# Attention, mixture of experts and Mish layer on one core: sorted rows transposed for the second expert alone, and the rest a turn later

## The chip, the core and the metric

The kernel runs on one core of a Trainium2 chip. The metric is device microseconds of one execution, lower is better. The engines are named as in the profile: PE is TensorE (PEld its weight loads), ACT is ScalarE, DVE is VectorE, POOL is GpSimd, SP is SyncE, which here only issues transfers. A name with a q behind it (SPq, PEq) is the engine's sequencer.

## What is computed

768 tokens pass through three layers, all in float32 in and out.

```python
# 1. attention, 8 heads of 64, masked to equal hash buckets (6 bits)
mask = q_bucket[:, :, :, None] == k_bucket[:, :, None, :]
attn_out = softmax(where(mask, scale * q @ k.T, -1e9)) @ v
# 2. mixture of experts: 8 experts, capacity 192, one expert per token
logits = x @ w_gate;  expert_idx = argmax(logits);  gate_w = softmax(logits)[expert_idx]
h = maximum(disp @ w1[e], 0)          # 512 -> 1024
y = h @ w2[e]                         # 1024 -> 512
out[token] = gate_w * y[slot of the token]
# 3. h * tanh(log1p(exp(h))), h = x @ w_in (512 -> 2048), then @ w_out (2048 -> 512)
```

With the inputs of this case the eight experts get 74, 76, 131, 118, 76, 79, 93 and 121 tokens. The third is the only one above 128.

## The kernel before

The program runs in three stages. Attention comes first, 48 units of 128 queries; it ends near 131 us. Then every token gets an expert and a slot, so that the tokens of one expert stand together ("sorted rows"). The experts stage follows, a loop of eight turns (`Fori(0, E)`, L948), one per expert. The Mish stage (L1088 and L1113) takes the rest. Each engine runs its own copy of the loop and waits on semaphores.

**One turn.** A turn of PE multiplies the expert's first weights (`wa`, the memory called `ring` in the profile) with transposed rows (`xs`, 512 features in four parts kd, a column per slot), in `first_layer` (L951, matmuls L959). It then multiplies the result with the second weights, split into a high and a low part (L1006). With at most 128 tokens it runs `narrow` (L992), 128 columns; with up to 144 `wider(MIDDLE)` (L1011). Which one runs is decided by a branch on the expert's count. Inside the first layer, behind the first block fc = 0, PE transposes the rows that the turn before has made (`turn_rows`, L982, matmuls L987), for which ACT has to have evicted `ysb` (L1314). The second weights are split during the turn: ACT rounds a quarter (`w2hi`, L1310), DVE subtracts (`w2lo`, L1647), four times.

**Where the rows come from.** For the first turn a matmul with a one-hot matrix (`hot`, L935) gathers the first expert's rows straight into PSUM banks 4 to 7, transposed; ACT (L1284) and DVE (L1620) evict them into `xs`. For all other turns POOL scatters all rows to `rows` in HBM in the order of their slots (six indirect DMAs, L665). SP waits for these (L517), reads them back to `xg` in three transfers (L520), and PE transposes them in 24 matmuls at the end of turn 0 (`rows_in`, L970, matmuls L978) into six banks. ACT (L1298) and DVE (L1634) evict three banks each.

**SP's order.** SP issues its transfers from one instruction stream: the three reads of `xg` first, then in a loop, for each next expert, the two halves of its first weights (L477, when PE has read the old ones, by the count `Hw`) and of its second weights (L481). Each half is 1 MB. `hold` (L412) is a wait, and L415 its line in the profile.

**POOL.** After the scatters POOL waits for all transposes (`xt`, L668) and the end of turn 1 (`Yw`, L669), and then splits the first ten blocks of the Mish weights, into memory that `hot` and `xg` lie in.

Of the kernel before, what the change touches and what calls it, by code (L numbers as in the profile page):

```python
# [31 lines left out]
P = 128  # L32
# [38 lines left out]
def attention_moe_mish(nc, kt, qt, vt, first, proj1, projs, foldw, w1, w2, w_in, w_out, cf, cb, out,  # L71
# [30 lines left out]
    with ExitStack() as ctx:  # L102
# [37 lines left out]
        mark = place("mark", [P, 5], F32)  # L140
# [53 lines left out]
        hot = place("hot", [P, NT, NARROW], F32)  # L194
        xg = place("xg", [P, NT, DM + 1], F32)
# [62 lines left out]
        for n in ["first_" + n for n in MISH_A + MISH_B] + ["wm" + str(f) for f in range(NS, KFF, 2)] + ["still", "c0", "c", "cr", "k0", "q00", "q01", "k1", "q1", "pj", "pj2", "qs", "cl", "passed_sp", "passed_gp", "rk0", "rk1", "rv0", "rv1", "ca", "cq", "cp", "pja", "pjb", "ah", "ab", "ao", "ak", "aq", "ka", "kl", "ks", "ch", "cc", "opsA", "opsB", "wa0", "wa1", "wb0", "wb1", "wi", "wo", "wi2", "wo2", "out",  # L258
                  "pjh", "pjl", "wg",
                  "S", "max", "P", "T", "hi", "lo", "PV", "OT", "os", "om", "xw", "fw", "fr", "lx", "lr", "pa", "pd", "vs", "rc", "tiny",  # L260
                  "g", "gex", "ohm", "lth", "gt", "gm", "gpos", "gst", "gkr", "hotr", "xga", "xgd", "perm", "tokc", "tokr", "prime", "si", "sc", "back", "back2", "wide", "xw0", "xw1", "xt", "xa", "xd",
# [11 lines left out]
        TURN = 4  # L273
# [53 lines left out]

        def load_bounds(engine, e):
# [7 lines left out]
        SHORT = WIDE // NEAR  # L336
        YB, YT, SLOW = 4, (5, 4), 6
        assert LAST_IN + 2 * NS + KF == 2 * KFF
        XT_BANKS = (0, 1, 2, 3, SLOW, SLOW + 1)
        FIRST_ROWS = 4  # L340
        assert FIRST_ROWS % NEAR == 0 and SHORT <= P
# [62 lines left out]
        def wide_slots(ks):  # L404

            return xs[:, ks, 0:WIDE].rearrange("q k (p t) -> q k t p", t=NEAR)

        def wide_tiles(bank):

            return ps[:, bank, 0:2 * WIDE].rearrange("q (k t p) -> q k t p", k=2, t=NEAR)  # L410
# [7 lines left out]
        def _(sp):  # L418
# [120 lines left out]
        def _(gp):  # L539
# [103 lines left out]
            nc.gpsimd.memset(mark[:, 0:1], 0.0).then_inc(s["xa"], 1)  # L643
            nc.gpsimd.memset(mark[:, 1:2], 0.0).then_inc(s["xd"], 1)
            nc.gpsimd.memset(mark[:, 2:3], 0.0).then_inc(s["Ha"], 2)
            nc.gpsimd.memset(mark[:, 3:4], 0.0).then_inc(s["Hd"], 2)
            nc.gpsimd.memset(mark[:, 4:5], 0.0).then_inc(s["ye"], 2)
# [20 lines left out]
            gp.wait_ge(s["xt"], 6)  # L668
# [22 lines left out]
        def _(pe):  # L691
# [238 lines left out]
            for t, kd in order:  # L930
# [4 lines left out]
                last = mm(ps[:, 4 + kd, 0:NARROW], xq[:, t, 2 * kd:2 * kd + 2, :].rearrange("p h d -> p (h d)"),  # L935
# [3 lines left out]
            pe.wait_ge(s["bnd"], 1)  # L939


            pe.wait_ge(s["bnd"], 1)
# [5 lines left out]
            with pe.Fori(0, E) as e:  # L948
                st, n_e = (pe.snap(x, min_val=0, max_val=T) for x in (at_r, many_r))

                def first_layer(W, fcs):  # L951

                    for fc in fcs:
                        if fc % (KF // 2) == 0:
                            pe.wait_ge(s[f"wa{2 * fc // KF}"], 16 * (e + 1))
                        for kd in range(KD):
                            if fc == 0:
                                pe.wait_ge(s["xd" if kd % 2 else "xa"], TURN * e + 2 + kd // 2)
# [3 lines left out]
                                      start=(kd == 0), stop=(kd == KD - 1), skip_group_check=True)  # L962
                        if fc % 2:
                            last.then_inc(s["Hw"], 1)

# [4 lines left out]
                def rows_in():  # L970

                    pe.wait_ge(s["back"], 16 * FIRST_ROWS // NEAR)
                    for b in XT_BANKS:
                        if b == SLOW:
                            pe.wait_ge(s["back2"], 16)
# [4 lines left out]
                        last.then_inc(s["xt"], 1)  # L980
# [11 lines left out]
                def narrow():  # L992

                    first_layer(NARROW, range(1))
                    turn_rows(e + 1)
                    first_layer(NARROW, range(1, KF))
# [14 lines left out]
                def wider(W):  # L1011

                    first_layer(W, range(1))
                    turn_rows(e + 1)
                    first_layer(W, range(1, KF))
# [16 lines left out]
                    with pe.If(e < 1):  # L1032
                        pe.wait_ge(s["ya"], 4)
                        pe.wait_ge(s["yd"], 4)
# [8 lines left out]
                with pe.If(e < 1):  # L1043
                    rows_in()
# [3 lines left out]
            with nc.body("pe_more", parent=turn, valid_engines=[pe.engine]):  # L1048
                with pe.If(e < 1):
                    pe.wait_ge(s["xa"], 3)  # L1050
                    pe.wait_ge(s["xd"], 3)
                    pe.wait_ge(s["back"], 16 * FIRST_ROWS // NEAR)
                    for kd in range(KD):
                        for t in range(NEAR):
                            at = WIDE * (kd % 2) + SHORT * t
                            last = mm(ps[:, 4 + kd // 2, at:at + SHORT], xg[0:SHORT, t, P * kd:P * kd + P],
                                      c32("ident")[0:SHORT, 0:SHORT], is_transpose=True, start=True, stop=True)
                    last.then_inc(s["wide"], 1)
                    pe.wait_ge(s["xw0"], 1)
# [734 lines left out]
```

## Time and profile before

| | us |
|---|---|
| median of 3 runs | 396.7 (396.29 to 397.35) |
| the profiled execution, its time | 397.59 |
| the profiled execution, its span | 395.8 |
| PE busy in it | 384.1 (97%) |
| attention and sorting, to the first turn | 0 to 141.2 |
| the eight turns | 141.2 to 256.3 |
| the Mish stage and the output | 256.3 to 395.8 |

The span is what the trace covers, and the execution's own time is 1.8 us more. PE is busy nearly all the time, so what PE waits for, and the clock it is granted, decide the time. A timeline row gives start, duration, engine, line and operation, out<-in and the count of instructions merged; square brackets hold the idle time before it and what ended it. Rows of PE overlap their neighbours because matmuls are pipelined. PE's count is two per matmul of float32 in the first layer (64 for 32 matmuls).

### The profile page before, as it was taken

The numbers are of one execution on the slowest core, as the hardware profiler recorded it, in microseconds if no ns is written. First come the engines' busy times: TensorE is split into PE (matmuls) and PEld (weight loads), VectorE is DVE, ScalarE is ACT, GpSimd is POOL, SyncE is SP. The second block draws the span as 40 slices with busy tenths as digits, with TensorE's granted clock in tenths as the row PEclk, the third lists the DMA queues.
The fourth block names the chain that finished last, engine by engine and source line by source line (L and its number), as shares of the span: only waits on it lengthen the run. The fifth ranks groups of instructions, "written<-read, shape, count | busy, mean of one in ns | idle before, by whom it ended". The sixth has DMA issues, their size and how long they took to land.

```text
span 395.8 us, 6807 instructions
## 1 busy us (share of the span) xinstructions
PE 384.1 (97%) x2384; PEld 348.2 (88%) x2386; DVE 281.6 (71%) x446; ACT 235.2 (59%) x454; POOL 116.1 (29%) x122
## 2 busy tenths in 40 slices
PE   8999999999999998899999999999999999999994
PEld 3688999999999897899998999899899988999883
DVE  4888998899998644430447744569899998876851
ACT  6969879869887544430444654467666665444631
POOL 1853543643810250039999400000000000000014
PEclk9999999999999999899999999999999999999999
DMA  8684934974903347896798889090000000000004
GB/s 284 227 200 106 268 82 131 291 152 111 417 34 146 127 159 292 332 368 238 263 365 286 296 333 357 0 317 5 0 2 0 2 0 2 1 0 2 0 4 162
DMA packets 16124, 62.93 MB, mean 159 GB/s; under 512 B 3008, under 2 KB 3904, under 8 KB 11488
## 3 DMA queue, kind: packets, MB, share of 16 engines
q1 hardware_dynamic: 14560, 58.61, 43.9%
q0 software_dynamic: 1024, 3.22, 2.2%
q10 hardware_dynamic: 512, 0.73, 0.5%
q8 instruction: 17, 0.28, 0.3%
q14 instruction: 11, 0.09, 0.1%
HBM read 49.89 MB, written 3.22 MB: 134 GB/s over the span
## 4 chain that ended last, share of the span: by engine, by line
PE 58%; DMA 3%; POOL 1%; issue 0%; SPq 0%; POOLq 0%; ACT 0%; DVE 0%; ACTq 0%
PE ps L1088 17%; PE ps L1113 16%; PE ps L959 13%; PE ps L1006 8%; DMA ring<-in_w 2%; PE ps L1027 2%; DMA rows<-xg,sloti 1%; PE ps L987 1%; POOL rows L665 0%; SPq L520 0%; POOLq L102 0%; POOL out L687 0%; DVE outs L1751 0%; ACT yh L1320 0%; ACT ysb L1314 0%
## 5 line engine op out<-in xcount | busy, mean ns | idle before, releaser
L959 PE MATMUL ps<-xs,ring 128*128 x512 | 61.9, 280 | 2.4 <-DMA ring<-in_w 2.4
L959 PEld LDWEIGHTS ps<-xs,ring 128*128 128x128 f32 x512 | 60.8, 195 | 3.1 <-issue 2.7
L1555 DVE TENSOR_TENSOR ptl<-ps,pth 128x384 fp32r<-128x384 f32 x96 | 49.0, 552 | 4.3 <-ACT pth L1246 3.7
L1246 ACT ACTIVATE pth<-ps 128x384 fp32r<-128x384 f32 x96 | 41.9, 491 | 16.0 <-PE ps L881 15.7
L1478 DVE TENSOR_REDUCE nmax<-ps 128x1 f32<-128x768 f32 x48 | 45.7, 955 | 4.9 <-PE ps L751 2.0
L683 POOL DMA_INDIRECT spare<-fold,toki x1 | 1.0, 1009 | 161.4 <-PE ps L1113 161.4
L751 PE MATMUL ps<-ops 128*128 128x384 f32 x192 | 44.4, 353 | 0.8 <-DMA ops<-qo 0.7
L1200 ACT ACTIVATE prob<-ps,nmax 128x768 f32<-128x768 f32 x48 | 43.5, 906 | 0.2 <-DVE nmax L1478 0.2
L1088 PE MATMUL ps<-yh,wih 128*128 128x384 f32 x128 | 43.0, 336 | 0.3 <-ACT yh L1320 0.3
L1088 PE MATMUL ps<-yh,wlow 128*128 128x384 f32 x128 | 42.8, 335 | 0.0
L1088 PE MATMUL ps<-yl,wih 128*128 128x384 f32 x128 | 41.9, 335 | 0.0
L1647 DVE TENSOR_TENSOR w2lo<-ring,w2hi 128x1024 fp32r<-128x1024 f32 x28 | 37.5, 1338 | 4.9 <-ACT w2hi L1310 4.7
L881 PE MATMUL ps<-cfs,prob 128*128 128x128 f32 x288 | 39.9, 273 | 0.7 <-DVE ptl L1555 0.7
L1113 PE MATMUL ps<-woh,gl 128*128 128x512 f32 x96 | 37.6, 392 | 0.0
L1113 PE MATMUL ps<-wlow,gh 128*128 128x512 f32 x96 | 37.6, 391 | 0.0
L881 PEld LDWEIGHTS ps<-cfs,prob 128*128 128x128 f32 x288 | 33.9, 140 | 4.0 <-DVE ptl L1555 2.1
L1113 PE MATMUL ps<-woh,gh 128*128 128x512 f32 x96 | 37.3, 389 | 0.0
L751 PEld LDWEIGHTS ps<-ops 128*128 128x128 f32 x192 | 33.6, 189 | 2.4 <-issue 1.7
L853 PE MATMUL ps<-pth,vs 128*128 128x384 f32 x90 | 34.2, 379 | 0.0
L1372 ACT ACTIVATE et<-ps 128x768 f32<-128x768 f32 (+1 forms) x19 | 13.4, 706 | 30.9 <-PE ps L1088 30.9
L853 PE MATMUL ps<-ptl,vs 128*128 128x384 f32 x90 | 30.3, 337 | 0.0
L1310 ACT ACTIVATE w2hi<-ring 128x1024 fp32r<-128x1024 f32 x28 | 29.4, 1050 | 0.1
(192 smaller groups left out, 782.9 us busy)
## 6 DMA issues: line engine op xcount, KB each, us to landing
ring<-in_w SPq DMA_DIRECT2D x32, 1024.0 KB, 4.8
wraw<-in_w_in SPq DMA_DIRECT2D x2, 1280.0 KB, 8.1
wraw<-in_w_out SPq DMA_DIRECT2D x2, 1280.0 KB, 10.8
ops<-kh SPq DMA_DIRECT2D x12, 192.0 KB, 6.0
ops<-qh SPq DMA_DIRECT2D x6, 384.0 KB, 8.2
xg<-rows SPq DMA_DIRECT2D x3, 513.0 KB, 4.9
raw<-in_vt SPq DMA_DIRECT2D x4, 384.0 KB, 5.3
wraw<-in_w_in SPq DMA_DIRECT2D x6, 256.0 KB, 4.4
```

The source lines that it names most:

```text
L751: last = mm(ps[:, b + c, 0:HALF], o[:, a, P * u:P * u + P], o[:, kk, c * HALF:c * HALF + HALF], start=(a == QA), stop=(a == QB), skip_grou ...
L853: last = mm(ps[:, OB, 0:HALF], vs[:, (m // 4) % 2, ch, (m // 2) % 2, :, :].rearrange("p a d -> p (a d)"), x[:, m % 2, ch, :, :].rearrange( ...
L881: last = mm(ps[:, tile_banks(n)[b], P * ch:P * ch + P], prob[:, n % 2, HALF * b + P * ch:HALF * b + P * ch + P], c32("ident"), is_transpos ...
L959: last = mm(ps[:, fc // 2, (fc % 2) * WIDE:(fc % 2) * WIDE + W], wa[:, 2 * fc // KF, kd, P * (fc % (KF // 2)):P * (fc % (KF // 2)) + P], x ...
L1006: last = mm(ps[:, YB, :], x[:, fc, :], w, start=(fc == 0 and n == 0), stop=(fc == KF - 1 and n == 2))
L1088: last = mm(ps[:, bank + c, 0:HALF], w[:, kd, :], y[:, kd, c * HALF:c * HALF + HALF], start=(n == 0), stop=(n == 3 * KD - 1))
L1113: last = mm(ps[:, t, :], g[:, f % 4, ts], w, start=(first and n == 0), stop=(final and n == 2), skip_group_check=True)
L1200: av(prob[:, n % 2, :].rearrange("p (c n) -> p c n", c=2), score_tile(n), ACT.Exp, bias=nmax[:, n % 4:n % 4 + 1], accum_out=rowsum[:, n:n ...
L1246: av(pth[:, (n // HT) % 2, HT * b:HT * b + HT, n % HT, :], ps[:, tile_banks(n)[b], 0:HALF].rearrange("p (a c) -> p a c", c=P), ACT.Copy).t ...
L1478: V.tensor_reduce(nmax[:, n % 4:n % 4 + 1], score_tile(n), AX.XY, ALU.max, negate=True).then_inc(s["max"], 1)
L1555: V.tensor_tensor(ptl[:, m2, HT * b:HT * b + HT, u, :], ps[:, tile_banks(n)[b], 0:HALF].rearrange("p (a c) -> p a c", c=P), pth[:, m2, HT ...
L1647: V.tensor_tensor(low[:, 2 * (b % 2):2 * (b % 2) + 2, :], wb[:, b // 2, 2 * (b % 2):2 * (b % 2) + 2, :], w2hi[:, 2 * b:2 * b + 2, :], ALU. ...
```

## The change

Between turn 0 and turn 1 only one window of 128 slots is read back and transposed, the one that begins at the second expert's first slot. All sorted rows are read back later, behind the second expert's weights in SP's order, and transposed at the end of turn 1 for turn 2 and those after it. The window's start is a run-time value: DVE computes it (`second_at`, at most 768 - 128), and SP, ACT and DVE load it into a register. The window is read into the memory of `hot`, which is free by then. The gather's banks change from 4, 5, 6, 7 to 4, 3, 6, 7. In the first layer the first two blocks are now multiplied with kd 0 and 1 first, then `turn_rows` comes, then kd 2 and 3 of them, then the other blocks; the waits for `xs` go with these two halves. A branch for a wide second or third expert changes too; with these counts only its `e != 1` branch around `turn_rows` and an empty one are run, in turn 2.

```diff
@@ SP @@
+            sp.wait_ge(s["bnd"], 2)
+            at_second = load_second(sp)
             sp.wait_ge(s["sc"], 16 * NT)
             sp.wait_ge(s["perm"], KD)
-            for g in range(0, NT, NEAR):
+            sp.dma_start(second, rows[bass.ds(at_second, P), 0:DM]).then_inc(s["back"], 16)
+            def sorted_rows(g):
                 sp.dma_start(xg[:, g:g + NEAR, :], rows[P * g:P * g + P * NEAR, :].rearrange(
-                    "(p t) x -> p t x", t=NEAR)).then_inc(s["back" if g < FIRST_ROWS else "back2"], 16)
+                    "(p t) x -> p t x", t=NEAR)).then_inc(s["back2"], 16)
...
                     second_weights(i + 1, half)
+                if i == 0:
+                    for g in range(0, NT, NEAR):
+                        sorted_rows(g)
@@ POOL @@
-            gp.wait_ge(s["xt"], 6)
+            gp.wait_ge(s["xt"], 2 + len(REST_BANKS))
@@ PE @@
+                def first_layer(W, turned=False):
+                    pe.wait_ge(s["wa0"], 16 * (e + 1))
+                    pe.wait_ge(s["xa"], e + 1)
+                    pe.wait_ge(s["xd"], e + 1)
+                    layer_part(W, range(2), range(KD // 2))
+                    if turned:
+                        with pe.If(e != 1):
+                            turn_rows(e + 1)
+                    else:
+                        turn_rows(e + 1)
+                    pe.wait_ge(s["xa"], TURN * e + 2)
+                    pe.wait_ge(s["xd"], TURN * e + 2)
+                    layer_part(W, range(2), range(KD // 2, KD))
+                    layer_part(W, range(2, KF // 2), range(KD))
+                    pe.wait_ge(s["wa1"], 16 * (e + 1))
+                    layer_part(W, range(KF // 2, KF), range(KD))
...
+                def second_rows(s_done):
+                    for kd in range(KD):
+                        last = mm(ps[:, SLOW + 2 * kd // KD, P * (kd % 2):P * (kd % 2) + P], second[:, P * kd:P * kd + P],
+                                  c32("ident"), is_transpose=True, start=True, stop=True)
+                        if kd % 2:
+                            last.then_inc(s_done, 1)
...
-                with pe.If(e < 1):
-                    rows_in()
+                with pe.If(e < 2):
+                    with pe.If(e < 1):
+                        pe.wait_ge(s["back"], 16)
+                        second_rows(s["xt"])
+                        pe.wait_ge(s["xd"], TURN + 2)
+                    with pe.Else():
+                        all_rows(s["xt"])
+                        pe.wait_ge(s["xa"], TURN + 3)
+                        pe.wait_ge(s["xd"], TURN + 3)
@@ ACT (DVE alike, with the other half and the banks 0, 6, 3) @@
+                def second_rows():
+                    act.wait_ge(s["xt"], 2)
+                    av(xs[:, KD // 2:KD, bass.ds(at_second, P)], second_tiles(SLOW + 1), ACT.Copy).then_inc(s["xa"], TURN)
+                def all_rows(s_ready, ready, s_part, s_all, many):
+                    for n, b in enumerate(REST_BANKS[1::2]):
+                        act.wait_ge(s_ready, ready + 2 * n + 2)
+                        done = av(many_slots(b), many_tiles(b), ACT.Copy)
...
@@ DVE, before the loop @@
+            V.tensor_scalar(second_at[:, :], ps[:, 2, 1:2], float(T - P), None, ALU.min).then_inc(s["bnd"], 1)
             for t in range(1, NT, 2):
                 V.tensor_scalar(xg[:, t, 0:DM], ...).then_inc(s["xgd"], 1)
+            dve.wait_ge(s["bnd"], 2)
+            at_second = load_second(dve)
```

`TURN` is 2 and `REST_BANKS` is (0, 1, 6, 2, 3, 7): `all_rows` on PE fills these banks in this order with four transposes each, DVE evicts 0, 6, 3 and ACT 1, 2, 7. Banks 0 and 1 and bank 6 hold kd 0 and 1.

## Rows read from the trace of the kernel before

**Rows 1.** The page's first line.

```profile
span 395.8 us, 6807 instructions
```

**Rows 2.** PE's timeline from turn 0 to turn 2's second layer.

```profile
141.16 1.12 PE L959 MATMUL ps<-xs,ring 128*128 x8
...
148.72 0.48 PE L1006 MATMUL ps<-w2hi,hsh 128*128 128x512 f32 x1
...
154.03 0.39 PE L1006 MATMUL ps<-w2hi,hsl 128*128 128x512 f32 x1
154.38 2.84 PE L978 MATMUL ps<-cfs,xg 128*128 128x128 f32 x24
159.66 1.56 PE L959 MATMUL ps<-xs,ring 128*128 x8 [2.44 <-DMA ring<-in_w]
...
168.90 0.48 PE L1006 MATMUL ps<-w2hi,hsh 128*128 128x512 f32 x1
...
174.46 1.14 PE L959 MATMUL ps<-xs,ring 128*128 x8
...
182.74 8.00 PE L1027 MATMUL ps<-hs,ring 128*128 128x144 f32 x64
```

**Rows 3.** PE's timeline, the beginnings of turns 5 and 6.

```profile
216.94 1.05 PE L959 MATMUL ps<-xs,ring 128*128 x8
...
230.01 1.05 PE L959 MATMUL ps<-xs,ring 128*128 x8
```

**Rows 4.** SP's timeline: issues of transfers, three reads first, then weights.

```profile
149.04 1.28 SPq L520 DMA_DIRECT2D xg<-rows  x3
150.44 1.11 SPq L477 DMA_DIRECT2D ring<-in_w  x2
151.79 0.82 SPq L481 DMA_DIRECT2D ring<-in_w  x2
165.66 3.90 SPq L477 DMA_DIRECT2D ring<-in_w  x2
```

**Rows 5.** DMA issues, size, us to landing: at 149.0, 150.4, 152.3 and 165.7.

```profile
xg<-rows SPq DMA_DIRECT2D x1, 513.0 KB, 3.7
...
ring<-in_w SPq DMA_DIRECT2D x1, 1024.0 KB, 9.0
...
ring<-in_w SPq DMA_DIRECT2D x1, 1024.0 KB, 14.5
...
ring<-in_w SPq DMA_DIRECT2D x1, 1024.0 KB, 4.8
```

**Rows 6.** Stretches: length, PE, PEld, DVE, ACT, POOL busy, granted clock, DMA share, GB/s.

```profile
151.00:152.00 1.00, 1.00 (x7) 0.81 (x6) 0.59 (x1) 0.00 (x0) 0.00 (x0) 1.00 0.92 365
...
157.00:158.00 1.00, 0.22 (x3) 0.00 (x0) 0.75 (x2) 0.50 (x1) 0.00 (x0) 1.00 1.05 442
...
161.00:162.00 1.00, 1.00 (x7) 1.00 (x6) 0.00 (x0) 0.23 (x1) 0.00 (x0) 0.50 1.08 459
...
256.00:257.00 1.00, 0.53 (x4) 0.20 (x2) 0.00 (x0) 0.65 (x2) 0.00 (x0) 1.00 0.00 0
```

**Rows 7.** Timelines of ACT and DVE: evictions and splits around turn ends.

```profile
154.46 0.66 ACT L1314 ACTIVATE ysb<-ps 128x256 f32<-128x256 f32 x2 [4.12 <-PE ps L1006]
...
177.65 0.41 ACT L1329 ACTIVATE hs<-ps 128x288 f32<-128x288 f32 x1 [1.05 <-PE ps L959]
...
150.37 1.23 DVE L1647 TENSOR_TENSOR w2lo<-ring,w2hi 128x1024 fp32r<-128x1024 f32 x1 [0.23 <-ACT w2hi L1310]
155.51 0.69 DVE L1634 COPY xs<-ps 128x512 f32<-128x512 f32 x1 [3.92 <-PE ps L978]
```

**Rows 8.** Groups by form on DVE: count, busy, mean ns of one.

```profile
L1654 DVE TENSOR_TENSOR yl<-ps,yh 128x256 f32 x14 | 5.4, 421 | 30.9 <-ACT yh L1320 30.9
```

**Rows 9.** DVE's scaling before the loop, and POOL's second scatter.

```profile
137.65 1.27 DVE L1616 TENSOR_SCALAR xg<-xq,gk 128x512 f32<-128x512 f32 x3
...
139.35 0.96 POOL L665 DMA_INDIRECT rows<-xg,sloti  x1 [0.30 <-issue]
```

More of the change, by code:

```diff
@@ L326, in wait_task_read, with load_second @@
                 e.wait_ge(s["pa"], PA * (g - 1) + t - 4 + 1)
+        def load_second(engine):
+            return nc.values_load_multi_w_load_instructions(
+                second_at[0:1, 0:1], engines=(engine.engine,), min_val=0, max_val=T - P,
+                skip_runtime_bounds_check_because="at most T - P by the minimum that is written there")[1][0]
         def load_bounds(engine, e):
@@ L402, in many_tiles, with second_tiles @@
             return ps[:, b, :].rearrange("q (k t p) -> q k t p", k=2, p=P)
[L404 to L410, printed above, removed]
+        def second_tiles(bank):
+            return ps[:, bank, 0:2 * P].rearrange("q (k p) -> q k p", k=2)
         def hold(e, passed, semaphore, value):
@@ L992, in narrow @@
                 def narrow():
[L994 to L996 removed]
+                    first_layer(NARROW)
                     pe.wait_ge(s["ya"], 2 * e + 2)
@@ L1011, in wider @@
                 def wider(W):
-                    first_layer(W, range(1))
-                    turn_rows(e + 1)
-                    first_layer(W, range(1, KF))
+                    first_layer(W, True)
                     pe.wait_ge(s["ya"], 2 * e + 2)
@@ L1048, in _ @@
             with nc.body("pe_more", parent=turn, valid_engines=[pe.engine]):
[L1049 to L1059, printed above, removed]
-                    pe.wait_ge(s["xw1"], 1)
+                with pe.If(e < 2):
+                    with pe.If(e < 1):
+                        pe.wait_ge(s["xa"], 2)
+                        pe.wait_ge(s["wide"], 16)
+                        for kd in range(KD):
+                            last = mm(ps[:, SLOW, P * kd:P * kd + P], xg[:, 0, P * kd:P * kd + P], c32("ident"),
+                                      is_transpose=True, start=True, stop=True)
+                        last.then_inc(s["xwt"], 1)
+                        pe.wait_ge(s["wider"], 1)
+                    with pe.Else():
+                        turn_rows(e + 1)
+                        pe.wait_ge(s["xa"], TURN + 2)
+                        all_rows(s["xr"])
+                        pe.wait_ge(s["xra"], 1)
+                        pe.wait_ge(s["xrd"], 1)
                 pe.br_cond(n_e < MIDDLE + 1, "pe_middle", "pe_wide")
@@ L1292, in _ @@
                 st, n_e = load_bounds(act, e)
-                def rows_in():
-                    for n, b in enumerate(XT_BANKS[0::2]):
-                        act.wait_ge(s["xt"], 2 * n + 1)
-                        av(many_slots(b), many_tiles(b), ACT.Copy).then_inc(
-                            s["xa"], 1 if b < SLOW else TURN * (E - 2) + 2)
+                def second_rows():
[5 more added lines that the diff above has]
+                        done = av(many_slots(b), many_tiles(b), ACT.Copy)
+                        if n == 0 and s_part is not None:
+                            done.then_inc(s_part, 1)
+                        if n == 2:
+                            done.then_inc(s_all, many)
+                def rows_in():
+                    with act.If(e < 2):
+                        with act.If(e < 1):
+                            second_rows()
+                        with act.Else():
+                            all_rows(s["xt"], 2, s["xa"], s["xa"], ALL_TURNS - TURN - 3)
                 def narrow():
```

116 lines of the change are left out of this document (63 added, 53 removed).

## The prediction, as it was made before the changed kernel ran

> **What bounds the kernel now.** I read the page first, then PE's timeline through the turns, and then, for the one place where PE stands still, what the transfers and the clock do there. The span is 395.8 us [rows 1]. PE runs from turn to turn without a hole, and a steady narrow turn takes 230.01 - 216.94 = 13.07 us [rows 3]; turn 0 takes 154.38 - 141.16 = 13.22 us up to its transposes [rows 2]. The exception lies between turn 0 and turn 1. After 24 transposes PE idles 2.44 us, and what ends it is a transfer into `ring`, the first half of the second expert's first weights [rows 2]. It was issued at 150.44, behind the three reads of sorted rows (149.04), and needed 9.0 us; the same transfer on idle queues needs 4.8 us [rows 4, 5]. In the stretches shown the DMA engines are 0.92 to 1.08 busy, at 365 to 459 GB/s [rows 6]. So the weights wait for 1.5 MB of rows, of which turn 1 reads a sixth, 128 of 768 slots.
>
> A second loss follows. PE's granted clock is 1.00 in the pause and 0.50 at 161 to 162, that is 1.2 GHz and not 2.4 [rows 6]. Turn 1's first layer takes 168.90 - 159.66 = 9.24 us where turn 0's takes 148.72 - 141.16 = 7.56 us [rows 2]: 1.68 us lost. From the first transpose (154.38) to turn 2's first matmul (174.46) pass 20.08 us [rows 2]. This stretch is what the change works on.
>
> **The stretch with the change, step by step.** (1) SP issues a read of 128 rows of 2 KB, 0.26 MB, at 149.04, since the scatters that it waits for stay. The first 513 KB read landed after 3.7 us [rows 5], so this one is there by 152.7 at the latest, and PE asks for it at 154.38. It costs nothing, with 1.7 us of cover.
>
> (2) The first weights go out two issues of about 0.45 us earlier, near 149.5. An idle queue gives 149.5 + 4.8 = 154.3 [rows 5]; 0.26 MB ahead of them at 365 GB/s [rows 6] is 0.7 us if nothing of it overlaps, so 154.3 to 155.0. The halves behind follow at 2.5 us each: from the first half's landing at 159.4 to the fourth's at 152.3 + 14.5 = 166.8 are three halves [rows 4, 5]. That puts the other three near 157, 159.5 and 162.
>
> (3) PE transposes four tiles in place of 24, and now waits for DVE's copy of the first two. Before, DVE's first copy began 155.51 - 154.38 = 1.13 us after the first transpose, behind eight of them [rows 2, 7]. A transpose takes 2.84 / 24 = 0.118 us [rows 2]; six fewer make 0.43 us. The copy has 128x256 elements, for which the nearest group of DVE shows 0.42 us [rows 8]. ACT's copy of the other half begins when its `ysb` evictions end, at 155.12 [rows 7], and is needed only behind the first four matmuls and `turn_rows`; it is covered. Sum: 0.85 us.
>
> (4) Behind this wait stand PE's own branches: two ends of conditionals, the loop's end, the choice of the path. Until now they ran under matmuls still queued; now PE's queue is empty. From below the cost is nothing: at 154.38 a conditional left only some 0.12 us between the last matmul (154.03, one every 0.23) and the first transpose [rows 2]. From above it is the 1.05 us that ACT sat between its last eviction of turn 1 and its first of turn 2, with the loop's end, a register load and three branches in it [rows 7]; ACT, not the matmul, was late there. PE's way has no load from memory behind the wait, so I take 0.4. Turn 1 then starts at 154.38 + 0.85 + 0.4 = 155.6, and its weights (154.3 to 155.0) are there. The Trainium skill (Advanced Engine Details and Errata, Control Flow Timing) gives about 51 ns for a plain branch and 108 ns for a compare-and-branch. No row here isolates one; the estimate from that page would be 0.3 to 0.5 us, so it would leave the sum where it is.
>
> (5) Turn 1 costs 13.2 us, like turn 0, if the clock holds. Its splits need the second weights in time. Turn 0's last split ends at 151.60, 2.9 us behind the second layer's start [rows 2, 7]; a quarter of the second layer is (154.38 - 148.72) / 4 = 1.4 us, so PE needs it at +4.2: slack 1.3 us. In turn 1 the second layer starts at 163.2. The fourth half lands at 162; two roundings and two subtractions of 1.05 to 1.23 us behind it end near 166.4, against a need at 167.4. The cover is 1.0 us.
>
> (6) At the end of turn 1 (168.8) come the 24 transposes that have moved. They aren't cheaper than before, but dearer: before, they ran while the weights were under way anyway, and now nothing hides their 2.8 us. PE then waits for DVE's second copy and ACT's first. DVE's third bank of transposes is there 1.6 us after the first, its copy takes 0.69 [rows 7], so the wait ends at 2.3 us, and with 0.4 of branches at 2.7: under the transposes. With 1.05 of branches it would be 3.35, or 0.55 more. The other copies end about 3.5 us in, while PE does four matmuls and `turn_rows` (0.9 + 0.45 us); nothing.
>
> (7) The three reads now follow the fourth half (162). At 300 to 400 GB/s, 1.58 MB end at 166 to 167.3; needed at 168.8. Turn 2's first weights are issued near 160.2, queue behind them and land at 168.6 to 169.9; needed at 171.6. The cover is 1.5 us on both. Turn 2's second weights are needed only at the second layer, 8.3 us later [rows 2].
>
> (8) Small things, at nothing: DVE's added minimum (about 0.2 us) stands ahead of the scalings that POOL's scatters wait for, but DVE begins them at 137.65 and POOL takes the second at 139.35, bound by its own issue [rows 9]. The register loads stand where SP, ACT and DVE wait anyway. POOL's splits of Mish weights begin when turn 1's last copies are done, so beside turn 2, as before. The matmuls and waits per turn are as many as before, in another order. Behind turn 2 everything hangs on PE and moves along.
>
> **Sum:** 20.08 - (0.85 + 0.4 + 13.2 + 2.8) = 20.08 - 17.25 = 2.8 us gained. With the ends of step 4 (nothing, or 1.05 twice) it is 1.6 to 3.3. In other words: 2.44 of waiting and 1.68 of half clock go, and 1.3 come back as a new pause.
>
> The profiled execution took 397.59, 0.9 above the median of 396.7. Against itself it would give 394.8, against the median 393.9. Part of the runs' spread may be that not every run pays the half clock; then the median has less to win. I take 394.2.
>
> **The rivals.** (A) The pause in front of turn 1 still brings the clock down. It lasts about 0.8 us against 2.44. For: one pause of 2.44 did it. Against: in 256 to 257 PE was busy for only 0.53 us and kept 1.00 [rows 6]. Price 1.7: 395.9. Chance 0.12. (B) One of the covers of 1.0 and 1.5 us in steps 5 and 7 is too thin, since the transfers of two stages now follow without a break; 1 us is lost: 395.2. Chance 0.10. (C) The stall only moves: turn 2's first weights land 2.4 us after the need, at 174, and the half clock comes with it, as before. Price 2.4 + 1.7 = 4.1: 398.3. It decides from a mean rate under 300 GB/s over the 7.1 MB since 150.4; the trace shows 5.8 MB landed by 166.8, 350 GB/s, slow reads included. Chance 0.05. (D) Slower: the first weights don't come earlier, because the reads were not what held them. Then turn 1 starts at 159.66 with the half clock as before, and the 2.8 us of step 6 are added without anything in return: 399.5. The point at which gain turns to loss is a start of turn 1 at 174.46 - 16.0 = 158.4. Against: 9.0 against 4.8 us for the same transfer. Chance 0.03.
>
> (E) The changed loop body leaves PE without code at one of the added branches, and the code comes through busy queues, at most like a weight transfer, 4.8 us: 399.0. In the trace no branch of the loop shows such a gap, but the code there is laid out otherwise. Chance 0.02. The Trainium skill (Runtime: NRT & Kernel Launch, Instruction fetch mechanics) says that a taken branch out of the two pages held stalls the engine until the target page is fetched; that speaks against added branches in the loop, and no row here shows such a stall.
>
> **How the numbers follow.** My forecast has 0.68, and the likeliest time is 394.2. Its own range is 393.3 (3.3 off the median) to 395.6. The range reaches over B and most of A to 396.3; C, D and E, 0.10, stay out. A measurement of this kernel can tell 0.3%, 1.2 us, from no change, so faster means under 395.5. Nearly all of the forecast and of B, and some of A: 0.80. The rest of A and B, and a small part of the forecast: 0.11. C, D, E: 0.09.
>
> **What would show it.** PE's turn 1 should start near 155.6, with an idle of about 0.8 us before it put down to DVE's copy (step 3, 4), not to a transfer into `ring`; if it is over 1.5, the branches cost more than the upper end. Clock 1.00 from 155 to 165 and a first layer of about 7.6 us (step 5). 24 transposes near 168.8, turn 2 at about 171.7, no idle before it (6, 7). A wait for `ring` or `xg` at either place is B or C. The prediction is wrong in its core if the first weights land after 156, or if later turns take over 13.1 us each.

## The result, and the profile after

The kernel got slower: 401.03 us median of five executions (399.28 to 402.03) against 396.5 (396.29 to 397.35), ratio 1.0104, interval 1.0082 to 1.0127. The forecast was 394.2 with a range up to 396.3. The five fall into two groups. Two have a mean granted clock of 0.999 and take 399.3 and 399.9 us; three have 0.994 or 0.995 and take 401.0 to 402.0. The profiled execution is the first, 399.28 with a span of 397.5, against 395.8 in [rows 1]. One later execution, of early_three, took 641.61 us at a mean granted clock of 0.558, where its nine others took 393.6 to 395.2, and no time or count below includes it.

PE's timeline of the changed kernel (start, busy us, line, operation, count, idle before and what ended it), which answers to [rows 2]:

```profile
141.26 1.13 PE L967 MATMUL ps<-xs,ring 128*128 x8
...
156.04 0.60 PE L999 MATMUL ps<-cfs,hot 128*128 128x128 f32 x4
158.66 1.15 PE L967 MATMUL ps<-xs,ring 128*128 x8 [2.02 <-issue]
...
171.82 2.78 PE L1010 MATMUL ps<-cfs,xg 128*128 128x128 f32 x24
175.86 1.24 PE L967 MATMUL ps<-xs,ring 128*128 x8 [1.25 <-ACT xs L1342]
```

There are three places to see. Turn 0 lasts 156.04 - 141.26 = 14.78 us, where it lasted 13.22. Before turn 1 stands an idle of 2.02 that no transfer ends, and before turn 2 one of 1.25 that wasn't there. Turn 1 itself takes 171.82 - 158.66 = 13.16.

The chain of work that ended last, in order of time, at both pauses:

```profile
156.20 0.45 PE ps L999 x4
156.65 0.26 issue
156.91 0.44 DVE xs L1694
157.35 1.31 issue
158.66 1.15 PE ps L967 x8
...
171.98 2.63 PE ps L1010 x24
...
174.70 0.64 ACT xs L1342
175.34 0.52 issue
175.86 1.24 PE ps L967 x8
```

DVE's copy ends at 157.35 and PE's first matmul comes 1.31 us later, with "issue" between them: the weights lie there, and nothing that the profile records is waited for. What PE's queue does in between is recorded line by line (line, engine, operation, duration in ns three times, start and end in us). Among eight control instructions are three compare-and-branches, at the end of the conditional (L1072), at the loop's end (L960) and at the choice of the path (L1066):

```profile
L1072 PEldq COMPARE_BRANCH  x1: 194/194/194, 157.4 to 157.4; - x1
L960 PEldq COMPARE_BRANCH  x1: 220/220/220, 157.7 to 157.7; - x1
L1066 PEldq COMPARE_BRANCH  x1: 68/68/68, 158.1 to 158.1; - x1
```

The other five are register and semaphore instructions of 36 to 80 ns, and none of the eight starts more than 0.2 us after the end of the one before. So the 1.31 us are a row of small instructions, and no single stall. At the second pause the chain names ACT's last copy, but the waits in the code are for ACT's first copy and DVE's second, and DVE's second is the later one:

```profile
173.33 0.69 DVE L1700 COPY xs<-ps 128x512 f32<-128x512 f32 x1 [0.18 <-PE ps L1010]
```

It ended at 173.33 + 0.69 = 174.02. Behind it stand five compare-and-branches. SP's issues, answering to [rows 4], and the landings, answering to [rows 5]:

```profile
149.20 0.35 SPq L527 DMA_DIRECT2D hot<-rows  x1
149.67 0.83 SPq L483 DMA_DIRECT2D ring<-in_w  x2
...
ring<-in_w SPq DMA_DIRECT2D x1, 1024.0 KB, 5.0
hot<-rows SPq DMA_DIRECT2D x1, 256.0 KB, 2.8
```

The read landed at 152.0 and the first weights at 149.67 + 5.0 = 154.7, both 1.3 us or more before turn 0 was over. The transfers did what the prediction said of them. The loss is elsewhere.

For the experiments I divide the stretch from turn 0's first matmul to turn 2's first matmul, by PE's timeline. From turn 2's first matmul to the end of the span it is 221.5 or 221.6 us in the profiles of the changed kernel, 221.0 or 221.1 in those with the waits inside, and 221.3 and 221.0 in the two of before. In us ("to turn 1" and "to turn 2" are the transposes and the pause behind them; where turn 1's part is 14.8, turn 1 ran partly at half clock, that is a granted clock of 0.50, 1.2 GHz):

| kernel | turn 0 | to turn 1 | turn 1 | to turn 2 | whole |
|---|---|---|---|---|---|
| before [rows 2] | 13.22 | 5.28 | 14.80 | 0 | 33.30 |
| after | 14.78 | 2.62 | 13.16 | 4.04 | 34.60 |
| again | 13.15 | 2.52 | 13.15 | 4.04 | 32.86 |
| waits_inside | 13.17 | 2.30 | 13.67 | 2.62 | 31.76 |
| before_again | 14.89 | 3.20 | 13.58 | 0 | 31.67 |
| again_two | 14.77 | 2.53 | 14.80 | 4.08 | 36.18 |
| inside_two | 14.63 | 1.07 | 13.15 | 2.62 | 31.47 |
| again_three | 13.16 | 2.61 | 13.14 | 4.07 | 32.98 |
| early_three | 13.18 | 1.07 | 13.15 | 2.62 | 30.02 |

### The profile page after: what moved, and what is told of

The parts are those of the page before. It is cut to its first block, busy times and chain, and to the rows that moved or that the text cites. A ratio compares the mean times of both kernels' runs of the same rounds, so it can differ in the third digit from the quotient of the medians.

```text
span 397.5 us, 6844 instructions
## 1 busy us (share of the span) xinstructions
PE 383.4 (96%) x2389; PEld 346.6 (87%) x2390; DVE 282.2 (71%) x448; ACT 234.7 (59%) x455; POOL 116.1 (29%) x120
## 4 chain that ended last, share of the span: by engine, by line
PE 88%; DVE 3%; ACT 3%; issue 2%; DMA 2%; POOLq 0%; POOL 0%; SPq 0%; ACTq 0%; DVEq 0%
PE ps L1126 17%; PE ps L1151 16%; PE ps L967 14%; PE ps L1036 9%; PE ps L865 7%; PE ps L763 7%; PE ps L893 7%; PE ps L1055 2%; PE ps L720 2%; PE ps L947 1%; PE ps L836 1%; ACT prob L1238 1%; PE ps L1019 1%; DMA eproj<-in_proj 1%; ACT pth L1284 1%
## 5 line engine op out<-in xcount | busy, mean ns | idle before, releaser
L967 PE MATMUL ps<-xs,ring 128*128 x512 | 60.7, 276 | 3.3 <-issue 2.0
L967 PEld LDWEIGHTS ps<-xs,ring 128*128 128x128 f32 x512 | 59.4, 191 | 4.1 <-issue 3.7
```

The lines of the kernel that those rows point to most:

```text
L967: last = mm(ps[:, fc // 2, (fc % 2) * WIDE:(fc % 2) * WIDE + W], wa[:, 2 * fc // KF, kd, P * (fc % (KF // 2)):P * (fc % (KF // 2)) + P], x ...
```

## The experiments

They ran in four batches of four kernels, each with its own runs of before. Two theories stood at first. By the first, PE's branches behind a wait that blocks cost what is missing. By the rival, it is what else is new: the order of work (the banks and the split first layer), or the loads of the second expert's address.

**First batch.** before took 396.18 here.

**again**: the changed kernel, no edit.

> The changed kernel once more, for a second trace. In its first trace turn 0 takes 14.78 us instead of 13.22, because ACT's first eviction of turn 0 (hsh) begins at 146.66, 2.9 us behind the matmuls that it waits for. If that comes from the code, ACT's idle time ahead of its first hsh is over 5 us again and turn 0 again takes 14.5 to 15 us. If it was chance, ACT begins near 143.8 and turn 0 takes 13.2 us. Either way PE should stand 1.3 us between the end of DVE's copy and turn 1's first matmul, and 1.2 us ahead of turn 2. Ratio to before 1.007 to 1.013.

Measured: 397.52, ratio 1.0046 (1.0026 to 1.0066). Slower again, but by 1.3 us and not by 4.5. Turn 0 took 13.15, and the pauses were the same two. So the pauses are the kernel's own; turn 0's extra 1.6 us is not.

**waits_inside**: PE's waits for the copies no longer stand at the turn's end, ahead of its branches, but in the next turn's first layer, on counters of their own.

```diff
@@ PE, first layer @@
-                    pe.wait_ge(s["xa"], e + 1)
-                    pe.wait_ge(s["xd"], e + 1)
+                    pe.wait_ge(s["xpa"], e + 1)
+                    pe.wait_ge(s["xpd"], 3 * e + 1)
...
@@ PE, end of turns 0 and 1 @@
                         second_rows(s["xt"])
-                        pe.wait_ge(s["xd"], TURN + 2)
                     with pe.Else():
                         all_rows(s["xt"])
-                        pe.wait_ge(s["xa"], TURN + 3)
-                        pe.wait_ge(s["xd"], TURN + 3)
...
```

> The waits for the evictions stand in the first layer of the turn that needs them, on counters of their own, and no longer at the end of the turn before; so PE's branches run while its matmuls still drain. Theory (the pauses are branches laid bare by a wait ahead of them): 1.3 us less in front of turn 1 and 1.2 us less in front of turn 2, so about 2.5 us faster than the changed kernel, ratio to before 1.001 to 1.007; if the half clock comes from the longer pause, it goes too and the ratio is below 1.0. Rival (the pauses are the copies and the transfers themselves): no change, the idle time is then put down to a copy, and the ratio stays at 1.010.

Measured: 395.2, ratio 0.9964 (0.9943 to 0.9986). 2.3 us below again, for the same work in the same order. The pause before turn 2 is gone (4.04 to 2.62, the bare transposes), and the one before turn 1 is now ended by the weights, by the chain of waits:

```profile
149.31 6.96 DMA ring<-in_w
156.28 0.22 issue
156.49 1.15 PE ps L967 x8
```

The transfer took 7.0 us here where it took 5.0 in the first profile. Turn 1 itself is 0.5 longer than in again, for the second weights are late too: ACT's first rounding of them in turn 1 waits for the transfer.

```profile
161.25 1.06 ACT L1362 ACTIVATE w2hi<-ring 128x1024 fp32r<-128x1024 f32 x1 [1.55 <-DMA ring<-in_w]
```

This kernel is no faster than before at full clock. Of the 22 executions of before in this batch the eight with a mean clock over 0.996 have a median of 395.1.

**old_order**: the first layer's old order and banks, with the moved reads kept.

```diff
-        GATHER = (4, 3, SLOW, SLOW + 1)
+        GATHER = (4, 5, SLOW, SLOW + 1)
...
-                    layer_part(W, range(2), range(KD // 2))
+                    pe.wait_ge(s["xa"], TURN * e + 2)
+                    pe.wait_ge(s["xd"], TURN * e + 2)
+                    layer_part(W, range(1), range(KD))
...
```

> The first layer in the old order (block 0 whole, then the transposes of the turned rows, then the rest) and the gather in the old banks 4 to 7; all else as in the changed kernel. Theory (the interleaved order or the new bank makes turn 0's first results late for ACT): turn 0 takes 13.2 us again, ACT begins at 143.8, 1.5 us less. Rival (it comes from the loads of the window's start, or from chance): turn 0 stays at 14.8 us. In front of turn 2 PE now waits for all copies, about 1 us more than the changed kernel.

Measured: 398.66, ratio 1.0063 (1.0042 to 1.0084), 1.1 above again. PE waited for 2.22 and 1.50 us at the two places and started turn 0 with a wait of 0.57 for DVE. The new order isn't the cause; it gains 1.1 us.

**loads_inside**: ACT's and DVE's loads of the second expert's address moved into turn 0's end (DVE's part; ACT's is alike).

```diff
             dve.wait_ge(s["bnd"], 2)
-            at_second = load_second(dve)
...
                 def second_rows():
 
+                    at_second = load_second(dve)
                     dve.wait_ge(s["xt"], 1)
```

> ACT and DVE load the window's start into a register only at the end of turn 0, not ahead of the loop; all else as in the changed kernel. Theory (the added load ahead of the loop makes ACT late in turn 0): ACT's first hsh begins near 143.8, turn 0 takes 13.2 us, 1.5 us less. Rival (the order of the first layer, or chance): turn 0 stays at 14.8 us. The load then stands in front of the copies of the window, where it costs 0.5 us or is hidden by the transposes.

Measured: 397.41, ratio 1.0031 (1.0008 to 1.0053), like again within the error. The rival falls as the cause of the pauses: from the end of DVE's copy (154.92) to PE's first matmul (156.14) it is 1.22 us here too. But the stretch is 32.51 us, 0.35 shorter than in again, since DVE's copy begins 154.50 - 153.99 = 0.51 us after the first transpose and not 0.87:

```profile
154.50 0.42 DVE L1694 COPY xs<-ps 128x256 f32 x1 [3.22 <-PE ps L999]
```

**Second batch.** before took 396.41 here.

**before_again**: before, no edit.

> The kernel before, unchanged, for a second trace of it. The prediction counted 1.68 us of half clock in turn 1 as lost in every run of it. If that holds, turn 1's first layer takes about 9.2 us here too, behind an idle of 2.4 us that a transfer into ring ends, and the later clock is 0.5 for a stretch. The other theory, that only some runs pay it: a first layer of 7.6 us, the same idle of about 2.4 us, and a span shorter by about 1.7 us (394.2). Ratio 1.000 by both.

Measured: 396.35, ratio 1.0001 (0.9988 to 1.0015). Neither of the two courses expected, but a third:

```profile
141.45 0.89 PE L959 MATMUL ps<-xs,ring 128*128 x6
142.96 0.48 PE L959 MATMUL ps<-xs,ring 128*128 x2 [0.63 <-DVE xs L1620]
...
156.34 2.78 PE L978 MATMUL ps<-cfs,xg 128*128 128x128 f32 x24
159.54 1.54 PE L959 MATMUL ps<-xs,ring 128*128 x8 [0.42 <-ACT xs L1298]
...
173.12 1.14 PE L959 MATMUL ps<-xs,ring 128*128 x8
```

Turn 0 is late here too (14.89), turn 1 starts at 159.54 where it started at 159.66 in [rows 2], and the idle has shrunk from 2.44 to 0.42. There is no half clock in these turns, and turn 2 starts at 173.12, earlier than with the short turn 0. So the 2.44 us idle of [rows 2] is slack for turn 0: when turn 0 is late, before loses nothing.

ACT's timeline shows how it is late. Its first eviction of turn 0, in before_again:

```profile
140.75 0.28 ACT L1284 ACTIVATE xs<-ps 128x128 f32<-128x128 f32 x1 [1.51 <-PE ps L935]
146.98 0.38 ACT L1305 ACTIVATE hsh<-ps 128x256 fp32r<-128x256 f32 x1 [5.95 <-PE ps L959]
```

In the profiled execution of before that eviction began at 143.64, after 2.90 of idle; in the changed kernel of the first result at 146.66, after 5.82:

```profile
143.64 0.38 ACT L1305 ACTIVATE hsh<-ps 128x256 fp32r<-128x256 f32 x1 [2.90 <-PE ps L959]
```

```profile
146.66 0.38 ACT L1360 ACTIVATE hsh<-ps 128x256 fp32r<-128x256 f32 x1 [5.82 <-PE ps L967]
...
153.20 0.47 PE L1036 MATMUL ps<-w2hi,hsh 128*128 128x512 f32 x1 [0.77 <-DVE hsl L1718]
```

PE's matmuls run on in the records meanwhile, but ACT sees their results some 3 us later than in the short course. Then DVE and ACT split the second weights late, and PE waits for them in the second layer. By ACT's idle ahead of this eviction, ten of the 18 profiles of this study have the short turn 0 (2.8 to 3.7 us) and eight the late one (5.8 to 6.0), and nothing lies between. The late eight are the first result's profile, all four of the second batch and three of the third.

**before_early**: before, with one issue moved.

```diff
+            hold(sp, s["passed_sp"], s["Hw"], 2)
+            first_weights(1, 0)
             sp.wait_ge(s["sc"], 16 * NT)
...
-                    hold(sp, s["passed_sp"], s["Hw"], 4 * i + 2 * half + 2)
-                    first_weights(i + 1, half)
+                    if i or half:
+                        hold(sp, s["passed_sp"], s["Hw"], 4 * i + 2 * half + 2)
+                        first_weights(i + 1, half)
```

> The kernel before with one issue moved: the first half of the second expert's first weights goes out when the first half of turn 0's first layer is done (near 146.8), ahead of the wait for the scatters and of the three reads; nothing else is changed. If the idle before turn 1 is due to the weights queued behind the reads, and PE's branches cost little there because matmuls cover them, turn 1 starts right behind the 24 transposes (157.2), 2.4 us earlier: about 393.9 against 396.4 (ratio 0.994), and the clock stays at 1.00. If the reads now come late (two of them share the engines with 0.5 MB of weights), the transposes of turn 0's end start up to 1 us later: 394.9.

Measured: 396.27, ratio 0.9998 (0.9980 to 1.0016). Turn 0 was late, the weights were no longer awaited, and nothing was gained: whole stretch 31.86 against 31.67.

**early_inside**: waits_inside with the same issue moved (the same edit of SP).

> waits_inside with the same issue moved: the first weights of turn 1 near 146.8 instead of 149.4. In waits_inside they landed 2 us behind turn 0's end and set turn 1's start at 156.49. If nothing else is late, turn 1 starts when the four transposes (154.7) and DVE's first copy (0.42, after 0.3 of idle) are through: near 155.4, 1.0 us earlier than there, 0.9974 of waits_inside, about 394.2 against 395.2. If PE's branches are still behind the last wait, 156.0 and 394.8.

Measured: 396.05, ratio 0.9991 (0.9977 to 1.0005). Turn 0 took 14.68, to turn 1 1.07, to turn 2 2.61. The pause before turn 1 is as expected, but behind a late turn 0.

**before_warm**: before, with ten matmuls on zeros behind the 24 transposes.

```diff
                     rows_in()
+                    keep_clock(10, 5)
```

> The kernel before with ten matmuls on a tile of zeros (128x512, 0.21 us each, into a free bank) behind the 24 transposes of turn 0's end, so that PE is busy while it waits for the weights; the weights come no earlier. If the half clock is paid in each run of before, this gains 1.7 us (394.7, ratio 0.9957). If the median run of before doesn't pay it, the ratio is 1.000 and only the slowest runs become rarer.

Measured: 396.96, ratio 1.0016 (0.9994 to 1.0039). Turn 0 was late, so little idle was left to fill; the filler delayed turn 1, which began 161.67 - 156.90 = 4.77 us after the first transpose where before_again had 3.20. The run doesn't settle the price of the half clock, since there was none to save.

**Third batch.** before took 395.86 here. The new theory: the changed kernel has lost the slack that hid a late turn 0.

**again_two**: the changed kernel, no edit.

> The changed kernel, unchanged, once more. The traces so far show two courses of turn 0 for both kernels: one of 13.2 us, in which ACT starts its first eviction 2.9 us after its last copy, and a late one of 14.7 to 14.9 us, in which that takes 5.8 to 5.9 us. Theory: before hides the late course, since its turn 1 starts at 159.5 with the weights either way; the changed kernel doesn't. Where the late course comes up in this batch, this takes 399 to 401 (ratio 1.007 to 1.010), turn 0 lasts 14.8 us; where it does not, 397.5 (ratio 1.004 or 1.005) and 13.2 us. If the course has nothing to do with it, the ratio is 1.0046 with either.

Measured: 400.5, ratio 1.0098 (1.0063 to 1.0132), with turn 0 at 14.77. The first result's ratio is back, and the late turn 0 with it. Not only the profiled execution is late: at a mean clock of 0.998 or more, two of the four here took 399.2 and 399.9, where those of again and again_three took 397.0 to 397.8. The profiled execution of this run is one of those with the half clock. PE's timeline, and the stretches (length, busy us of PE, PEld, DVE, ACT, POOL, granted clock, DMA share, GB/s):

```profile
158.89 1.15 PE L967 MATMUL ps<-xs,ring 128*128 x8 [1.92 <-issue]
...
173.69 2.78 PE L1010 MATMUL ps<-cfs,xg 128*128 128x128 f32 x24
177.77 1.24 PE L967 MATMUL ps<-xs,ring 128*128 x8 [1.30 <-ACT xs L1342]
...
159.00:160.00 1.00, 1.00 (x9) 1.00 (x10) 0.00 (x0) 0.00 (x0) 0.00 (x0) 0.97 0.98 410
160.00:161.00 1.00, 1.00 (x7) 1.00 (x6) 0.00 (x0) 0.39 (x2) 0.00 (x0) 0.50 1.08 442
```

The clock falls from 2.4 to 1.2 GHz 1.1 us after the new pause, and turn 1 takes 14.80 where it took 13.16 after a pause of the same length in the first profile: 1.64 us.

**inside_two**: waits_inside, no edit.

> waits_inside, unchanged, once more, to be compared with again_two in one batch. It should be 2.3 us under it as in the first batch if the two pauses behind the copies are what it saves, whichever course turn 0 takes. Against before: 395.2 (0.9964) with the short turn 0, 397 (1.001) with the late one.

Measured: 396.11, ratio 0.9997 (0.9980 to 1.0014). 4.4 us below again_two, more than the 2.3 expected. The chain shows what is left of the pause, 0.12 in place of 1.21 or 1.31 between copy and matmul:

```profile
156.89 0.44 DVE xs L1691
157.33 0.12 issue
157.45 1.15 PE ps L967 x8
```

And the half clock doesn't come up in this kernel: of the 48 executions with the waits inside (this kernel and the early ones) none has a mean granted clock under 0.997, of the 21 of the unedited changed kernel eight have 0.994 or 0.995. The pause's length alone doesn't decide it. waits_inside had 1.70 us of idle in its profile and none of nine, loads_inside 1.56 and one of ten, old_order 2.22 and none of four.

**early_two**: early_inside, no edit.

> early_inside, unchanged, once more, to be compared with inside_two in one batch. Theory: with the short turn 0 the first weights land 2 us behind its end, and issuing them at 146.8 instead of 149.4 brings turn 1 forward by 0.9 to 1.1 us: 394.2 (0.9939 of before). With the late turn 0 they have landed anyway, and the two kernels are equal within 0.4 us.

Measured: 396.12, ratio 1.0001 (0.9991 to 1.0012). Equal to inside_two, as expected with a late turn 0.

**plain_writes**: POOL's indirect writes made direct, so the tokens stay unsorted.

```diff
-                gp.indirect_dma_start(out=rows[:, :], out_offset=bass.IndirectOffsetOnAxis(ap=sloti[:, t:t + 1], axis=0),
-                                      in_=xg[:, t, :], in_offset=None).then_inc(s["sc"], 16)
+                gp.dma_start(rows[P * t:P * t + P, :], xg[:, t, :]).then_inc(s["sc"], 16)
```

> The changed kernel with POOL's six indirect writes of the rows replaced by six direct writes of the same size to unsorted places (it leaves out the sorting of the tokens, so the experts see other rows; the work on them is the same). The late course of turn 0 lies beside these six writes. If they hold back PE's signals, or the start of the kernel's turns, turn 0 lasts 13.2 us here where again_two has 14.8, and the kernel gains about 1.5 us more than the writes' own end brings. If the late course comes from elsewhere, turn 0 is as long as in again_two. Either way SP's read of the second rows goes out up to 3 us earlier, which alone is worth nothing for turn 1's start, since its weights wait for turn 0's first layer.

Measured: 398.21, 2.3 below again_two on the same chip and, at a mean clock of 0.998 or more, 397.4 to 398.6 against 399.2 and 399.9, ratio 1.0052 (1.0034 to 1.0069) to before. Turn 0 took 13.09, and ACT was on time:

```profile
144.72 0.38 ACT L1359 ACTIVATE hsh<-ps 128x256 fp32r<-128x256 f32 x1 [2.87 <-PE ps L966]
```

The four profiles of this batch are three late turns with the indirect writes and one short turn without them. The direct writes are also issued sooner, by 142.4 where the indirect ones take until 145.9 in again_two, so the kind of write and its time aren't told apart.

**Fourth batch.** before took 395.32 here.

**writes_later**: the indirect writes held back until half of turn 0's first layer is done.

```diff
+            gp.wait_ge(s["Hw"], 2)
             for t in range(NT):
```

> The changed kernel with POOL's six indirect writes held back until half of turn 0's first layer is done (Hw 2, near 145), some 7 us later than before. Where turn 0 takes its late course (14.8 us, again_three in this batch) and the writes themselves hold PE's signals, the gather's last copies and turn 0's first layer are on time here (first eviction 2.9 us after ACT's last copy and not 5.9) and the hold, if any, appears later. If it comes from something else at this place, ACT's first eviction is as late as in again_three. The rows then arrive about 6 us late, near 160, so turn 1 starts later and the time is 4 to 6 us above again_three.

Measured: 405.69, ratio 1.0254 (1.0221 to 1.0287), from two executions. Turn 0 was short in again_three as well, so this tells nothing of the late course. The rows came late: PE waited 6.00 us for `hot`.

**again_three**: the changed kernel, no edit.

> The changed kernel, unchanged, as the measure for this batch: 397.5 with the short turn 0 (13.2 us), 400.5 with the late one (14.8 us).

Measured: 397.39, ratio 1.0062 (1.0028 to 1.0096), turn 0 at 13.16. As with again: short turn 0, 397.4.

**early_two_before**: before_early, no edit.

> before_early, unchanged, once more: the kernel before with only the first weights issued ahead of the reads. With the late turn 0 it gave nothing (0.9998). If this batch has the short turn 0, the weights are there when the 24 transposes end, and turn 1 starts 2.0 to 2.4 us earlier than in before, with no half clock: about 394 (ratio 0.994). With the late turn 0 again 1.000.

Measured: 395.07, ratio 0.9982 (0.9961 to 1.0002). With a short turn 0 the earlier weights brought no gain that can be told either, since they took bandwidth from the rows that PE transposes next. Their reads landed after 5.9 us (median) where they took 4.9 in before, and PE waits for them:

```profile
155.88 1.97 PE L981 MATMUL ps<-cfs,xg 128*128 128x128 f32 x16 [1.02 <-DMA xg<-rows]
158.58 1.09 PE L981 MATMUL ps<-cfs,xg 128*128 128x128 f32 x8 [0.74 <-DMA xg<-rows]
160.09 1.47 PE L962 MATMUL ps<-xs,ring 128*128 x8 [0.41 <-ACT xs L1301]
```

So the change's idea, to read only the 128 rows that turn 1 needs, does what it is for: weights early and all rows early don't go together.

**early_three**: early_inside, no edit.

> early_inside, unchanged, once more. With the short turn 0: turn 1 starts about 14.2 us after turn 0 (13.2, four transposes, and a pause of 0.5), turn 2 at 30.0 us after it where waits_inside had 31.8: 393.5 to 394.2 (ratio 0.993 to 0.995). With the late turn 0: 1.000 as in the last batch.

Measured: 394.34, ratio 0.9964 (0.9950 to 0.9978), 3.05 below again_three. PE's timeline:

```profile
154.69 0.60 PE L1002 MATMUL ps<-cfs,hot 128*128 128x128 f32 x4
155.76 1.15 PE L970 MATMUL ps<-xs,ring 128*128 x8 [0.47 <-DVE xs L1694]
...
168.91 2.78 PE L1013 MATMUL ps<-cfs,xg 128*128 128x128 f32 x24
171.53 1.15 PE L970 MATMUL ps<-xs,ring 128*128 x8
```

The whole stretch is 30.02 us, 0.5 below the 30.5 that the prediction's steps give (13.22 + 0.85 + 0.4 + 13.2 + 2.8). This kernel is faster than both where turn 0 is short, and even with before (0.9991, 1.0001) and 4.4 us faster than the changed kernel where it is late. The gain over before in this batch is not the half clock alone: the 18 of 21 executions of before with a mean clock over 0.996 have a median of 395.2.

## Why the prediction was wrong

The steps that concerned transfers were right. Those that concerned PE at a wait, and what before really loses, were not.

By its steps the stretch would have taken 13.22 + 17.25 = 30.47 us. In again_two it took 36.18, 5.71 more: 1.55 in turn 0, 1.28 up to turn 1 (steps 3 and 4), 1.60 in turn 1 (the half clock, rival A) and 1.28 up to turn 2 (step 6). The prediction's sum is a gain of 2.8 and the result a loss of 4.5, 7.3 apart. The 1.6 that are left are the half clock of [rows 2], counted as a loss in before, which most of its executions outside the first batch don't show.

**Steps 1, 2, 5 and 7, right.** The read landed at 152.0 (said: by 152.7), the first weights at 154.7 (154.3 to 155.0). Turn 1 took 13.15 and 13.16 us (13.2) with no wait for the second weights, and no wait for `xg` or `ring` stands before turn 2. Rivals B to E didn't come up in the changed kernel: no transfer was waited for, and PE's control instructions follow each other with no gap over 0.2 us (E). The covers of step 2 and step 5 are thin all the same. In waits_inside the first weights landed at 156.3, past the prediction's own mark of 156, and the second weights cost turn 1 0.5 us.

**Step 4 is the one that failed, for the size.** It took the branches behind the wait at 0.4 us and gave 1.05 as an upper bound, from ACT's branches. They cost 1.31 and 1.21 in the chains, 0.12 with the waits inside, so 1.1 to 1.2 us. A bound from another engine was no bound for PE: its compare-and-branches lasted 194, 220 and 68 ns there, and five more instructions stood between them, which the step didn't count. The Trainium skill (Advanced Engine Details and Errata, Control Flow Timing) has 108 ns for a compare-and-branch, from which I estimated 0.3 to 0.5; the three records and the 1.1 to 1.2 us in all disagree, and the measurement decides.

**Step 3** was short by 0.46: DVE's copy ends 157.35 - 156.04 = 1.31 after the first transpose, not 0.85, since it begins 0.87 after it and not 0.43. With the waits inside it begins 0.51 after it (156.89 - 156.38), and in loads_inside too, where DVE's load of the address is moved. So 0.36 of the 0.46 go with either edit. Why wasn't found. Steps 3 and 4 together: 2.52 to 2.62 against 1.25.

**Step 6 failed where it called the branches hidden.** It let DVE's second copy end at 2.3 us, under the transposes; it ended at 174.02 - 171.82 = 2.20. From there to turn 2's first matmul it is 1.84 us, not 0.4. Even the version with 1.05 was too small. 4.04 against 2.8, so 1.2 more; waits_inside takes them all back (2.62).

**The sum was made against a loss that before doesn't always have.** The prediction credited 1.68 us for the half clock and asked itself whether all runs pay it. In the first batch 14 of 22 executions of before have a mean clock of 0.996 or less; in the three others 10 of 75. And where turn 0 is late, the idle of 2.44 isn't there: before_again, 31.67 us and full clock. (Seven of the 54 executions of before in the two batches with late profiles still have 0.996 or less; no trace shows where.) Against 31.6 to 31.7 the changed kernel's 32.9 is 1.2 us of loss, and up to 0.5 more lies behind turn 2's first matmul (221.5 us against 221.0 to 221.3). In the medians, 397.52 - 396.18 and 397.39 - 395.32 are 1.3 and 2.1.

**What the prediction didn't have at all** is the late turn 0. It took the 2.44 us of idle as a loss to be won. It is also the cover for a turn 0 that is about 1.6 us late in eight of 18 profiles. Take it away, and the lateness shows: 2.9 us over before_again in the first profile (34.60 - 31.67), and 4.5 with the half clock in again_two (36.18 - 31.67). In terms, for three of the first result's five executions, with before_again standing for before and again_two for the half clock: turn 1 starts 17.4 us after turn 0 in place of 18.1 (-0.7), it is itself 0.4 shorter than in before_again (13.16 against 13.58), the transposes and the pause before turn 2 add 4.0, and the half clock 1.6, together 4.5. That is 401.0 - 396.5. Which course before itself took beside that result isn't known, but its time hardly depends on it.

**Rival A had the right mechanism** and got 0.12. The half clock does come after the new pause, in 8 of 21 executions by their mean clock. The pause is 1.9 to 2.0 us and not 0.8, and with the 0.47 of inside_two and the early kernels it didn't come in 39. Its price was right (1.64 measured, 1.7 said).

## What to carry to other kernels

A wait put in front of an engine's branches costs the branches as well, if nothing queued is left to run under them. Put it behind them, at the first instruction that needs the data. And an idle that a transfer ends isn't a gain until one knows what else it hides: here a stage before it that is late in eight of 18 profiles. A loss seen in one profile should be checked against the spread of the clock in the other runs before it is counted.

## What the runs showed of the hardware

- PE needed 1.2 to 1.3 us from a blocking wait's end, through the conditional's end, the loop's end and the choice of the path, to its first matmul, and 1.84 with two more compare-and-branches at the second place. With the wait behind them the gap before the first matmul is 0.12, and before turn 2 there is none.
- Turn 0 has two courses, 13.1 to 13.3 and 14.6 to 14.9 us (waits for rows at its end left out). The four batches ran on four chips; within a batch the four profiles had the same course, but for plain_writes. In the late one ACT sees PE's results some 3 us late, in the time in which POOL's indirect writes are issued (138.3 to 145.9 in again_two, ACT's eviction at 147.1), and the one kernel without indirect writes was short in a late batch. That the writes take part rests on that one kernel; how they hold back what ACT sees, and why only on some chips, is open. Writes at another time were tried only in a batch with the short course.
- The half clock after a pause of about 2 us isn't certain: the turns 1 that begin at 158.66 (the first result) and 158.89 (again_two) start after 2.02 and 1.92 of idle, the first ran on at 2.4 GHz, the second at 1.2.
